# Attention rows stored as half rows in 16 DMAs instead of 80, with a ring of 18 steps and two gathers per expert tile

## The reference

```python
# attention: batch 8, heads 8, seq 576, head_dim 64
kv  = einsum('bhsd,bhse->bhde', k, v)
out = einsum('bhsd,bhde->bhse', q, kv)
out = out / sqrt(mean(out*out, -1) + 1e-6) * g_norm
x = out.transpose(0, 2, 1, 3).reshape(4608, 512)
# experts: 8 of them, 512 -> 1024 -> 512, one per token
logits = x @ w_gate + modality_bias[modality_id]
e = argmax(logits); gate = softmax(logits)[e]
y[t] = gate[t] * (relu(x[t] @ w1[e[t]]) @ w2[e[t]])
# gated layer: 512 -> 1536 -> 512
out = (sigmoid(y @ w_gate2) * (y @ w_val)) @ w_out
```

## Time and profile before

| | us |
|---|---|
| three runs | 1542.50, 1549.01, 1551.57 |
| median | 1549.01 |
| profiled execution | 1545.89 |
| its span | 1544.1 |
| last normalisation of attention (`xb`) begins | 174.3 |
| first `up` matmul of an expert tile | 209.8 |
| mean granted clock of TensorE | 0.96 |
| TensorE busy | 1414.0 (92%) |
| VectorE busy | 862.4 (56%) |
| DMA to `x_rows`: 64 of 128 KB, 16 of 64 KB | |
| DMA from q, k, v: 8 each of 1152 KB | |
| DMA of weights to `raw`: 64 of 512 KB | |

### The profile page before, as it was taken

One profiled execution on the slowest core, in us unless ns is written; L12 is line 12 of the kernel. 1 busy time (PEld: TensorE's weight loads), 2 busy tenths in 40 slices (PEclk: granted clock), 3 DMA queues, 4 the chain that ended last, 5 costly groups with the idle time before them and its releaser, 6 DMA issues.

```text
span 1544.1 us, 25404 instructions
## 1 busy us (share of the span) xinstructions
PE 1414.0 (92%) x8566; PEld 1162.9 (75%) x8567; DVE 862.4 (56%) x1420; ACT 435.5 (28%) x766; POOL 253.8 (16%) x328
## 2 busy tenths in 40 slices
PE   4555469999999999988999999999999999999997
PEld 3444448887888888877777888888888888888886
DVE  3454756366645666244776556655575555755551
ACT  4554212222222222223442113321143211422122
POOL 0052512223223323221211001000010000100001
PEclk9777679999999999998999999999999999999999
DMA  9775334255424555419997434094332743234411
GB/s 333 256 265 164 83 103 149 66 169 171 149 94 126 154 156 145 101 34 287 347 302 190 181 143 170 5 263 149 143 123 94 217 150 143 75 139 164 153 62 41
DMA packets 121037, 241.67 MB, mean 157 GB/s; under 512 B 18039, under 2 KB 72311, under 8 KB 114816
## 3 DMA queue, kind: packets, MB, share of 16 engines
q1 hardware_dynamic: 83200, 199.29, 39.5%
q0 software_dynamic: 10560, 29.69, 6.0%
q10 hardware_dynamic: 27200, 11.64, 2.9%
HBM read 179.44 MB, written 51.73 MB: 150 GB/s over the span
## 4 chain that ended last, share of the span: by engine, by line
PE 82%; DVE 5%; issue 5%; DMA 4%; ACT 2%; SPq 1%; ACTq 0%; DVEq 0%; POOL 0%; POOLq 0%
PE ps L1508 29%; PE ps L1488 17%; PE ps L1435 14%; PE ps L1457 13%; PE ps L1444 2%; PE ps L1373 2%; PE ps L1360 2%; DMA graw<-in_moe_w_val 1%; PE ps L1478 1%; DMA mixes<-mix 1%; PE ps L1337 1%; DMA vt<-in_v 1%; ACT qp L715 0%; DMA xs<-x_rows,tok_x 0%; DVE mix L1200 0%
## 5 line engine op out<-in xcount | busy, mean ns | idle before, releaser
L1508 PE MATMUL ps<-a_hi,st 128*128 128x512 f32 x1344 | 421.5, 389 | 0.8 <-DVE u L1282 0.8
L1508 PEld LDWEIGHTS ps<-a_hi,st 128*128 128x128 f32 x1344 | 252.3, 188 | 54.0 <-DVE a_lo L1243 1.2
L1488 PE MATMUL ps<-wo,shi 128*128 128x512 f32 x864 | 272.2, 396 | 5.7 <-DVE slo L1252 5.0
L1508 PE MATMUL ps<-a_lo,st 128*128 128x512 f32 x672 | 261.4, 389 | 0.0
L1435 PE MATMUL ps<-ew,xhi 128*128 x640 | 202.7, 398 | 13.6 <-DVE xlo L1112 12.3
L1457 PE MATMUL ps<-ew,hhi 128*128 x640 | 197.2, 389 | 1.3 <-DVE hlo L1128 1.3
L1488 PEld LDWEIGHTS ps<-wo,shi 128*128 128x128 f32 x864 | 163.0, 189 | 45.4 <-issue 4.9
L1488 PE MATMUL ps<-wo,slo 128*128 128x512 f32 x432 | 170.7, 395 | 0.0
L660 POOL DMA_INDIRECT out<-ot,out_tok x36 | 36.0, 999 | 719.2 <-ACT ot L817 713.4
L1435 PEld LDWEIGHTS ps<-ew,xhi 128*128 128x128 f32 x640 | 118.1, 190 | 37.8 <-issue 14.9
L1508 PEld LDWEIGHTS ps<-a_lo,st 128*128 128x128 f32 x672 | 126.2, 188 | 26.2
(11 more groups left out here) (217 smaller groups left out, 1805.1 us busy)
## 6 DMA issues: line engine op xcount, KB each, us to landing
st<-mixes SPq DMA_DIRECT2D x48, 1792.0 KB
raw<-in_moe_w SPq DMA_DIRECT2D x64, 512.0 KB, 5.6
mixes<-mix SPq DMA_DIRECT2D x24, 512.0 KB, 8.2
xg<-xs ACTq DMA_DIRECT2D x160, 64.0 KB, 2.2
kt<-in_k SPq DMA_DIRECT2D x8, 1152.0 KB, 10.1
vt<-in_v SPq DMA_DIRECT2D x8, 1152.0 KB, 12.7
qt<-in_q SPq DMA_DIRECT2D x8, 1152.0 KB, 9.6
mixes<-gv SPq DMA_DIRECT2D x12, 768.0 KB, 6.4
```

Source lines behind the costliest of these rows:

```text
L1488: last = mm(ps[:, 4 + m, :], s[:, rows], wo[f // 2][:, w, f % 2], start=(f == 0 and w == 0 and s is shi[slot]), stop=(f == GC - 1 and s is ...
L1508: last = mm(bank_of(f, idx), st[f % 2][:, at:at + 128], x[:, idx, k, :], start=(k == 0 and w == 0 and x is a_hi), stop=(k == 1 and w == 1))
```

## The change

The DRAM tensor `x_rows` now has a half row per row: 9216 rows of 256 floats, ordered by batch, partition and `j`. A batch's steps of one partition lie next to each other, so a store takes all 128 partitions and 4 or 5 steps at once, in pieces of 4 or 5 KB per partition (`PIECE`): 16 stores. The ring `xb` has 18 steps, two batches. The number that is sorted is no longer the token's but the *seat* of its first half, `1152 b + 9 r + j`; the second half's seat is 576 further. A tile's gather becomes two, one for each half, from two columns of `seat_of`. The gates' list needs token numbers, which DVE works out from the seats in five more dependent steps (`tok_step`).

POOL makes the hot rows of the first two groups, the first half of the third (8) and of the last (4); DVE makes the others (`own_hots`): 8 of the third group at the end of its `place_part`, 4 of the last where it made 8. Tile 0's four quarter loads are split between ACT and SP (`load_quarters`). `xb` takes 18 instead of 8 KB per partition; several early constants now share their place with `hot`, and `hot_q` and `moved` lie over the k and v buffers. The rest of the diff renames `tok_` to `seat_`. Context lines are thinned out, and indentation is cut by four.

```diff
@@ -64,7 +64,8 @@
-RING = 8
+RING = 2 * J
+PIECE = [(0, 4), (4, J)]
@@ -73,6 +74,7 @@
+OWN = {g: (GROUPS[g][0] + GROUPS[g][1] // 2) // 2 for g in (LAST - 1, LAST)}
@@ -84,14 +86,14 @@
-x_rows = nc.dram_tensor("x_rows", [N, D], F32, kind="Internal").ap()
+x_rows = nc.dram_tensor("x_rows", [2 * N, HALF], F32, kind="Internal").ap()
-x_v = x_rows.rearrange("(b r j) (n x) -> b n r j x", r=R, j=J, n=2)
+x_v = x_rows.rearrange("(b p j) x -> b p j x", p=128, j=J)
...
@@ -446,7 +442,13 @@
     def hot_row(engine, k, part):
-        return engine.tensor_scalar(hot[:, k, part], across[:], spot_r[:, k:k + 1], tok_part[:, part, k:k + 1], ALU.is_equal, ALU.mult)
+        return engine.tensor_scalar(hot[:, k, part], across[:], spot_r[:, k:k + 1], seat_part[:, part, k:k + 1], ALU.is_equal, ALU.mult)
+    def load_quarters(engine, t, quarters):
+        engine.wait_ge(sorted_in, 32 * t.n + 32)
+        for g in quarters:
+            engine.dma_start(xg[32 * g:32 * g + 32, t.p], xs[:, 128 * g:128 * g + 128]).then_inc(x_in[t.p], 16)
@@ -459,16 +461,11 @@
-        def store(o):
-            sp.wait_ge(x_normed, 2 * o + 2)
-            at, b, j = 2 * o % RING, 2 * o // J, 2 * o % J
-            for n in range(2):
-                part = slice(R * n, R * n + R)
-                if spans_two(o):
-                    sp.dma_start(x_v[b, n, :, j], xb[part, at]).then_inc(x_out[o % (RING // 2)], 16)
-                    sp.dma_start(x_v[b + 1, n, :, 0], xb[part, at + 1]).then_inc(x_out[o % (RING // 2)], 16)
-                else:
-                    sp.dma_start(x_v[b, n, :, j:j + 2], xb[part, at:at + 2]).then_inc(x_out[o % (RING // 2)], 16)
+        def store(b, n):
+            j0, j1 = PIECE[n]
+            sp.wait_ge(x_normed, J * b + j1)
+            at = J * (b % 2)
+            sp.dma_start(x_v[b, :, j0:j1], xb[:, at + j0:at + j1]).then_inc(x_out[b % 2][n], 16)
@@ -485,11 +482,13 @@
-            o = s - LAG_NORM - 1
-            if o >= 0:
-                store(o)
+            for b in range(BATCH):
+                for n in range(2):
+                    if s == (J * b + PIECE[n][1] - 1) // 2 + LAG_NORM + 1:
+                        store(b, n)
         for unit in range(EARLY, UNITS):
+        load_quarters(sp, Tile(0, 0), (2, 3))
@@ -581,19 +580,20 @@
-            nc.gpsimd.iota(tok_i[R * n:R * n + R], [[SEQ, BATCH], [1, J]], base=0, channel_multiplier=J).then_inc(iota_made, 1)
+            nc.gpsimd.iota(seat_i[R * n:R * n + R], [[2 * SEQ, BATCH], [1, J]], base=0, channel_multiplier=J).then_inc(iota_made, 1)
-        for g, (c0, m) in enumerate(GROUPS[:LAST]):
+        for g, (c0, m) in enumerate(GROUPS):
-            for k in range(c0 // 2, (c0 + m) // 2):
+            for k in range(c0 // 2, OWN[g] if g in OWN else (c0 + m) // 2):
                 for part in range(2):
-        for n in range(RING // 2):
-            pool.wait_ge(x_out[n], stored(S - RING // 2 + n))
+        for b in range(2):
+            for n in range(2):
+                pool.wait_ge(x_out[b][n], 16 * BATCH // 2)
         def when(sem_, count):
@@ -603,11 +603,12 @@
-            nc.gpsimd.tensor_copy(tok_x[:], tok_of[:, bass.ds(t.n, 1)]).then_inc(aimed, 1)
+            nc.gpsimd.tensor_copy(seat_x[:], seat_of[:, :, bass.ds(t.n, 1)].rearrange("p n a -> p (n a)")).then_inc(aimed, 1)
-            nc.gpsimd.indirect_dma_start(
-                out=xs[:], out_offset=None, in_=x_rows,
-                in_offset=bass.IndirectOffsetOnAxis(ap=tok_x[:], axis=0)).then_inc(sorted_in, 16)
+            for n in range(2):
+                nc.gpsimd.indirect_dma_start(
+                    out=xs[:, HALF * n:HALF * n + HALF], out_offset=None, in_=x_rows,
+                    in_offset=bass.IndirectOffsetOnAxis(ap=seat_x[:, n:n + 1], axis=0)).then_inc(sorted_in, 16)
         def gather_gate(t):
@@ -622,13 +623,13 @@
-        pool.wait_ge(list_made, 1)
+        pool.wait_ge(list_made, 2)
         for n in range(2):
         pool.wait_ge(gates_out, 16)
-        pool.wait_ge(list_made, 4)
+        pool.wait_ge(tok_step, 6)
         def tile_step(i, c):
@@ -748,12 +749,9 @@
-        def load_x(t):
+        def load_x(t, quarters=(0, 1, 2, 3)):
-            act.wait_ge(sorted_in, 16 * t.n + 16)
-            for g in range(4):
-                act.dma_start(xg[32 * g:32 * g + 32, t.p],
-                              xs[:, 128 * g:128 * g + 128]).then_inc(x_in[t.p], 16)
+            load_quarters(act, t, quarters)
         def xhi_of(t):
@@ -777,7 +775,7 @@
-        load_x(Tile(0, 0))
+        load_x(Tile(0, 0), (0, 1))
...
@@ -1000,6 +998,15 @@
+            if g == LAST - 1:
+                own_hots(g)
+        def own_hots(g):
+            dve.wait_ge(spot_made, g + 1)
+            for k in range(OWN[g], (GROUPS[g][0] + GROUPS[g][1]) // 2):
+                for part in range(2):
+                    last = hot_row(nc.vector, k, part)
+            last.then_inc(last_hot_made, 1)
@@ -1022,11 +1029,12 @@
-                if o >= RING // 2:
-                    dve.wait_ge(x_out[o % (RING // 2)], stored(o - RING // 2))
                 for jj in range(2):
+                    b, j = (2 * o + jj) // J, (2 * o + jj) % J
+                    if b > 1 and j in (PIECE[0][0], PIECE[1][0]):
+                        dve.wait_ge(x_out[b % 2][0 if j == 0 else 1], 16 * (b // 2))
                     nc.vector.tensor_tensor(
-                        xb[:, 2 * o % RING + jj].rearrange("p (g h i) -> p h g i", g=2, h=PAIRS),
+                        xb[:, (2 * o + jj) % RING].rearrange("p (g h i) -> p h g i", g=2, h=PAIRS),
@@ -1049,20 +1057,25 @@
-        dve.wait_ge(spot_made, len(GROUPS))
-        for k in range(GROUPS[LAST][0] // 2, KP):
-            for part in range(2):
-                last = hot_row(nc.vector, k, part)
-        last.then_inc(last_hot_made, 1)
+        own_hots(LAST)
         nc.vector.memset(split_to[:], UNITS // 2).then_inc(exp_asked, 1)
         dve.wait_ge(pe_order, 1)
-        nc.vector.tensor_copy(tok_of[:], ps[:, 6, 0:NT]).then_inc(list_made, 1)
+        nc.vector.tensor_copy(seat_of[:, 0], ps[:, 6, 0:NT]).then_inc(list_made, 1)
+        nc.vector.tensor_scalar(seat_of[:, 1], ps[:, 6, 0:NT], float(SEQ), None, ALU.add).then_inc(list_made, 1)
+        routed = steps[0]
-        nc.vector.tensor_copy(tok_b[:], ps[:, 6, 64:64 + NT]).then_inc(list_made, 1)
+        steps[0] = 0
+        chain(tok_step, nc.vector.tensor_copy(seat_b[:], ps[:, 6, 64:64 + NT]))
+        chain(tok_step, nc.vector.tensor_scalar(tok_b[:], seat_b[:], 7, None, ALU.logical_shift_right))
+        chain(tok_step, nc.vector.tensor_scalar(tok_b[:], tok_b[:], 57.0, None, ALU.mult))
+        chain(tok_step, nc.vector.tensor_scalar(tok_b[:], tok_b[:], 9, None, ALU.logical_shift_right))
+        chain(tok_step, nc.vector.tensor_scalar(tok_b[:], tok_b[:], float(SEQ), None, ALU.mult))
+        chain(tok_step, nc.vector.tensor_tensor(tok_b[:], seat_b[:], tok_b[:], ALU.subtract))
+        steps[0] = routed
@@ -1405,11 +1418,13 @@
             if k == GROUPS[LAST][0] // 2:
-                pe.wait_ge(last_hot_made, 1)
+                pe.wait_ge(hot_made, LAST + 1)
+            if k in OWN.values():
+                pe.wait_ge(last_hot_made, 1 if k == OWN[LAST - 1] else 2)
             for part in range(2):
         last.then_inc(pe_order, 1)
-        pe.wait_ge(list_made, 2)
+        pe.wait_ge(list_made, 3)
```

More of the change, by code:

```diff
@@ L181, in moe_program @@
     past = att("past", [128, KP, E - 1], F32)
-    moved = att("moved", [128, KP, E - 1], F32)
     step = att("step", [128, E - 1], F32)
     spot_t = att("spot_t", [128, KP], F32)
+    early = Place(att.at)
+    bias_b = early("bias_b", [128, T, E], F32)
+    mid_raw = early("mid_raw", [128, BATCH, 2 * J], I32)
+    mid = early("mid", [128, 2, T], F32)
+    ident_i = early("ident_i", [128, 128], I32)
+    tri_i = early("tri_i", [R, 128], I32)
+    across_i = early("across_i", [128, 128], I32)
+    turn_i = early("turn_i", [128, 4, 32], I32)
+    fold_b = early("fold_b", [128, 128], F32)
+    wg = early("wg", [128, DC, E], F32)
     hot = att("hot", [128, KP, 2, 128], BF16)
-    hot_q = att("hot_q", [128, KP, NT], BF16)
     mb = att("mb", [128, 2, E], F32)
-    mid_raw = att("mid_raw", [128, BATCH, 2 * J], I32)
-    mid = att("mid", [128, 2, T], F32)
     bias = att("bias", [128, T, E], F32)
-    bias_b = att("bias_b", [128, T, E], F32)
     pri_i = att("pri_i", [128, E], I32)
-    tok_i = att("tok_i", [128, T], I32)
+    seat_i = att("seat_i", [128, T], I32)
     base_i = att("base_i", [128, E], I32)
@@ L229, in moe_program @@
     r_ex = route("r_ex", [128, T, E], F32)
+    moved = route("moved", [128, KP, E - 1], F32)
+    hot_q = route("hot_q", [128, KP, NT], BF16)
     r_den = route("r_den", [128, T], F32)
@@ L322, in moe_program @@
         acc_made = sem("acc_made")
-        x_out = [sem(f"x_out{n}") for n in range(RING // 2)]
+        x_out = [[sem(f"x_out{b}_{n}") for n in range(2)] for b in range(2)]
```

(16 more changed lines are left out.)

21 lines of the change are left out of this document (8 added, 13 removed).

## The result

The changed kernel takes 1538.7 us (median of 14 runs, 1533.0 to 1542.5) against 1548.9 for the kernel before (14 runs): ratio 0.9938 [0.9924, 0.9952], 10 us faster where 27 were forecast. The profiled execution is the lowest of the 14, 1533.0 us with a span of 1530.8, so from profile to profile the gain is 12.9 us.

The account below looks back on a forecast made before the run. In the front part it took VectorE's `xb` waits on stores, 26.6 us, as the bound. Terms -26.6 - 2.5 + 2.1 - 1.2 + 0.15 + 2.0 - 1.3 = -27.4 took 1549.0 to 1521.6 us; range 1514 to 1535.

Parts of the forecast that it names:

- The ring: Attention stage: with 18 steps, VectorE's five waits of `xb` on a store vanish, -26.6 us (bounds 0 to -26.6).
- What is late next? The loads. ... So no new stall: 0: Attention stage: q, k and v still land before they are wanted, DMA work filling 78%; cost 0, +6 at worst.
- The clock, -2.5: Attention slots after each stall: TensorE's granted clock drops less once stalls go, -2.5 us (bounds 0 and -5).
- rival C: Attention stage: stalls go but their time is passed on, matmuls and copies waiting, clock low; 1543 to 1549, chance 0.06.
- The stores' rate: Stores of `xb`: merged 4 and 5 KB pieces taken at 365 GB/s, 1 KB pieces at 213; no gain summed.
- Routing: End of routing: VectorE's 8 third-group hot rows add +2.1 us on the path; GpSimd's 4 last-group rows are covered.
- The gather pair, +2.0: Start of the tiles: a second gather costs its issue time, +1.0 us, twice on the path, +2.0.
- The tiles: Expert stage: the second gather of 38 more tiles stays covered within the 11.9 us between gathers; cost 0.
- Rival D: Expert tiles: the second gather costs more than its cover in each tile; slower, 1551 or 1582, chance 0.05.
- B: Attention stage: the loads become the bound; 1528, or 1535 if q is late too; chance 0.15.

Follow-up runs that it names:

- e2_light: Changed kernel with q, k and v loads cut to 16 columns of one head pair from the third batch on; first to last `xb` 119.3 us.
- e6_warm: Changed kernel with one extra matmul per slot where TensorE would wait for `qp`; 1540.2 us, a single execution.
- e3_twice: Changed kernel with each of the 16 stores issued a second time to an unread tensor, 9.4 MB more; 1542.6 us, ratio 0.996.
- e7_two_gathers: Kernel before with the 18-step ring and each tile's gather split in two; 80 stores, old routing; 1539.0 us, ratio 0.9929.
- e4_pool: Changed kernel with all 16 hot rows of the third group made on GpSimd again; 1536.3 us, ratio 0.9912.
- the ring alone: Kernel before with only the 18-step ring and its SBUF places; 80 stores, one gather, old routing; 1530.4 us, ratio 0.9886.

## Why the prediction was wrong

- **The ring: right.** All five waits of `xb` on a store are gone in every kernel with 18 steps, and none came back, even with twice the stores.
- **"What is late next? The loads. ... So no new stall: 0": this step failed**, and it is the prediction's error. The stage missed by 15.9 us, of which 2.5 are the clock's term. Its reasoning on the loads' data was right: the engines had room (queue 1 at 72.1% in 0 to 147 us, where 78% was estimated) and no engine waits for q or k. The question was put too narrowly. Besides data, the same DMA engines carry TensorE's instructions, and the burst of K^T V is nearly 300 records in 3 us. With the stalls of `xb` gone, TensorE runs out of instructions more often: 9.9 us of gaps in the bursts for 1.9, 12.2 for 6.1 with the turns of `qp`. That the stalls had given the supply time to catch up is the reading of this; it fits, but no run delays TensorE in another way to test it. The trace of before has two of these gaps in its bursts, 1.56 us at 27.76 and the one in this row, at the very place where the changed kernel has its gap at 63.23 (57 records in the row behind it in both), and 4.2 us ahead of a turn of `qp`. The prediction mentions none of them.

```profile
67.84 1.08 PE L1373 MATMUL ps<-vt,kt 64*64 64x64 f32 x57 [0.34 <-issue]
```

- What is shown: the traffic on the DMA engines costs the stage 19.5 us (e2_light), the gaps sit at fixed positions of the instruction stream (e6_warm), they grow with traffic (e3_twice), and every one ends 1.2 to 1.6 us after an instruction packet has landed, in all profiles. No record shows TensorE's sequencer waiting, but nothing else in the traces ends these gaps. What is not shown is the whole sum: the gaps themselves account for some 6 of the stage's 15.9 us (12.2 less 6.1), and ScalarE's wait for the burst grew by 9.7. Of the 19.5 us of e2_light some 5.6 lie outside that wait; they weren't split further.
- **The Trainium skill** (Runtime: NRT & Kernel Launch, Instruction fetch mechanics) says that each engine's sequencer fetches its instructions by DMA in blocks of 16 KiB and that this fetch is hidden, since the sequencer dispatches more slowly than it is filled. The traces have the block (19 packets, 0.31 MB in the stage), but not the hiding: they have gaps of up to 4.35 us where the DMA engines are full. The measurement decides.
- **The clock, -2.5: wrong.** The clock did not recover with the stalls gone (mean 0.73 and 0.81 in 24 to 162 us, 0.80 before), and the stage took 138.8 and 138.0 us at these two. That its pace is the latency from engine to engine, as rival C's "for" had it, fits but is not shown.
- **The stores' rate: right in direction, and worth nothing that can be measured.** In 125 to 165 us, where queue 1 carries stores alone, it moved 2.77 MB in 17.0% of 40 us, 407 GB/s, where the earlier trace rows give 213 for 1 KB pieces and the prediction took 365. The Trainium skill's 512 B for the line rate (DMA: Bandwidth & Descriptors, Specifications) is not borne out: pieces of 1 KB were far from the rate of the larger ones. Yet 80 stores with two gathers (e7_two_gathers, 0.9929) and 16 with two (the change, 0.9938 and 0.9916) are the same, though the two also differ in the hot rows and in tile 0's quarters.

```profile
q1 hardware_dynamic: 656, 2.77, 17.0%
```

- **Routing: right.** VectorE's 8 rows cost 2.34 us at 157.43, and ScalarE's `rms` waits 5.18 behind them, 2.04 more than in e4_pool (3.14), where 2.1 was forecast; the earlier trace rows have 3.59. GpSimd's four were covered, as forecast.

```profile
157.43 2.34 DVE L445 TENSOR_SCALAR hot<-across,spot_r,seat_part 128x128 bf16<-128x128 f32 x8
161.69 0.30 ACT L683 ACTIVATE rms<-ssum,eps 128x8 f32<-128x8 f32 x1 [5.18 <-DVE ssum L1044]
170.75 3.71 POOL L445 TENSOR_SCALAR hot<-across,spot_r,seat_part 128x128 bf16<-128x128 f32 x4 [7.19 <-DVE spot_r L996]
```

- **The gather pair, +2.0: undersized.** From the first gather's issue to the landing of the second, the first pair takes 4.28 us (178.53 to 182.81) where the earlier trace rows have 3.65 for one; the second pair takes 5.75 (187.35 to 193.10), where one gather with the ring alone takes 3.51: +2.9 by the change, +3.1 by e7_two_gathers. In the second pair the second half lands 4.48 us after its issue, later than a whole gather does; in the first pair it took 2.78. The Trainium skill's fit (DMA: Bandwidth & Descriptors, Anatomy of one DMA) with fixed parts that don't overlap gave +4 for the two pairs; the trace lies midway between that estimate and mine. Whether e7_two_gathers pays more beyond the start, some 4 us by ratios whose intervals overlap, stays open.

```profile
178.53 1.19 POOL xs L609
...
180.03 2.78 DMA xs<-x_rows,seat_x
...
187.35 0.75 POOL xs L609
...
188.62 4.48 DMA xs<-x_rows,seat_x
```

- **The tiles: the cover held.** Rival D did not come: first gathers of tiles come 12.02 us apart in the steady state (11.9 in the earlier trace rows), and TensorE waits for no tile after the first.

```profile
284.25 0.96 POOL L609 DMA_INDIRECT xs<-x_rows,seat_x  x1 [0.79 <-POOL seat_x L606]
...
296.27 0.96 POOL L609 DMA_INDIRECT xs<-x_rows,seat_x  x1 [0.79 <-POOL seat_x L606]
```

- **The rivals.** B gave 1528 to 1535 from data that comes late; the place (the DMA engines) was right, the mechanism not, and the result lies beyond its range. C ("their time is passed on") came nearest in kind, at 1543 to 1549, but its means were the clock and the latency of matmuls and copies. Its chance of 0.06 looks too small afterwards: that released time runs into the next limit deserved more than one named case. The measured 1538.7 lies between the ranges of B and C, in neither.

## What to carry to other kernels

Before costing a removed stall at its full length, look for what else caught up during it. An `issue` gap inside a dense burst of tiny matmuls, at full DMA engines, is a sign of such a debt: set its end beside the instruction packets of the trace, and price it by making the loads tiny in one experiment. Spreading the burst over idle slots won 8.5 us here, not because the gaps got shorter in sum, but because less was waiting behind them. And try the parts of a bundle one by one: here the ring alone was at least as good as the bundle (clearly better than one of its two measurements), merging the stores brought nothing that can be measured, and splitting a gather in two cost more than its issue.

## What the runs showed of the hardware

- TensorE can run out of instructions: with the data queue at 64 to 79% of the DMA engines in 23 to 162 us, and at 97.2% around one gap, gaps of 0.3 to 4.4 us stood at the same few places of the program in the kernels with the same TensorE program, and nearly vanished (0.76 us in all) with the queue at 29.6%. Each of the 63 gaps ended 1.2 to 1.6 us after a 16 KB packet of the instruction queue had landed.
- The second of two indirect DMAs of 128 half rows, issued 1.27 us behind the first, landed 4.5 us after its issue in the second pair of two kernels; in their first pairs the second took 2.8 us; a single one of twice the bytes took 3.5 to 3.65.
- Stores in pieces of 4 to 5 KB moved at 407 GB/s, in pieces of 1 KB at 213.
